# A fused attention and MLP kernel: one attention unit leaves the prologue and is worked through beside the first MLP steps

## The reference

```python
q_d = q.reshape(B, H, Sd, 4, D).mean(axis=3)          # the same for k_d, v_d
out_d = sm_attn(q_d, k_d, v_d)                        # softmax attention, 144 x 144
out_up = np.repeat(out_d, 4, axis=2)
mask = np.abs(pos[:, None] - pos[None, :]) < 4        # local attention
out_local = softmax(where(mask, scale * q @ k.T, -1e9)) @ v
x = (out_up + out_local)                              # 2304 tokens x 512
h = x @ w_in;  x = (h - np.tanh(h)) @ w_out           # 512 -> 2048 -> 512
h = x @ w2_in; out = (h * np.cos(h)) @ w2_out
```

## Time and profile before

| | |
|---|---|
| three runs | 918.26, 919.24 and 924.06 us, median 919.24 |
| the profiled execution | 918.26 us, span from the first to the last instruction 916.1 us |
| TensorE busy in the span | 903.7 us (99%) |
| DVE, ACT, POOL busy | 522.8, 376.0, 146.4 us |
| granted TensorE clock | 1.00 over the span |
| DMA | 59.57 MB, of it 20.45 MB in the first 90 us |

### The profile page before, as it was taken

How to read it: one execution, slowest core, us unless ns; L and a number is a source line. 1 busy time by engine, 2 the same in 40 slices (tenths; PEclk the granted TensorE clock), 3 DMA queues, 4 the chain that set the end, 5 groups by cost and what they waited for, 6 DMA issues and landing times.

```text
span 916.1 us, 15863 instructions
## 1 busy us (share of the span) xinstructions
PE 903.7 (99%) x6264; PEld 838.9 (92%) x6264; DVE 522.8 (57%) x1071; ACT 376.0 (41%) x1055; POOL 146.4 (16%) x167
## 2 busy tenths in 40 slices
PE   8899999999999999999999999999999999999998
PEld 6689999999999999999999999999999999898997
DVE  5733544444445434433334787777777777777775
ACT  6744443443344334422232444443443434443433
POOL 5587400200000100000079820000000000000000
PEclk9999999999999999999999999999999999999999
DMA  9692012821004600301134501001001000000000
GB/s 297 234 297 65 1 58 75 184 71 47 1 34 132 164 1 1 105 1 35 60 114 138 161 1 35 35 1 35 35 1 35 35 1 1 35 1 1 36 1 34
DMA packets 24637, 59.57 MB, mean 65 GB/s; under 512 B 2292, under 2 KB 5492, under 8 KB 24564
## 3 DMA queue, kind: packets, MB, share of 16 engines
q1 hardware_dynamic: 22212, 50.01, 15.9%
q0 software_dynamic: 2352, 8.55, 5.2%
HBM read 49.12 MB, written 9.44 MB: 64 GB/s over the span
## 4 chain that ended last, share of the span: by engine, by line
PE 96%; DMA 2%; DVE 1%; ACT 1%; issue 0%; POOL 0%; POOLq 0%
PE ps L488 44%; PE ps L533 22%; PE ps L514 22%; PE ps L406 2%; DMA qk<-qkx_in 2%; PE ps L446 1%; PE ps L457 1%; PE ps L415 1%; PE ps L389 1%; PE ps L424 1%; PE ps L430 1%; PE ps L401 1%; ACT ps L595 0%; DVE x L789 0%; DVE ps L737 0%
## 5 line engine op out<-in xcount | busy, mean ns | idle before, releaser
L488 PE MATMUL ps<-xh,wi_hi 128*128 128x384 f32 x768 | 261.9, 341 | 2.2 <-DVE gl L830 2.2
L488 PE MATMUL ps<-xh,wi_lo 128*128 128x384 f32 x768 | 258.0, 336 | 0.0
L488 PE MATMUL ps<-xl,wi_hi 128*128 128x384 f32 x768 | 257.3, 335 | 0.0
L488 PEld LDWEIGHTS ps<-xh,wi_hi 128*128 128x128 f32 x768 | 144.2, 188 | 9.4 <-DVE gl L830 2.5
L488 PEld LDWEIGHTS ps<-xl,wi_hi 128*128 128x128 f32 x768 | 144.3, 188 | 4.0
L488 PEld LDWEIGHTS ps<-xh,wi_lo 128*128 128x128 f32 x768 | 144.1, 188 | 0.0
L635 ACT ACTIVATE gh<-rem 128x384 fp32r<-128x384 f32 x96 | 50.5, 526 | 213.6 <-PE ps L533 141.7
L822 DVE TENSOR_TENSOR ps<-ps,fn 128x384 f32<-128x384 f32 x96 | 54.2, 565 | 144.3 <-ACT fn L623 143.4
L514 PE MATMUL ps<-gh,wo_hi 128*128 128x384 f32 x384 | 132.3, 345 | 0.0
L514 PE MATMUL ps<-gl,wo_hi 128*128 128x384 f32 x384 | 128.5, 335 | 0.0
L514 PE MATMUL ps<-gh,wo_lo 128*128 128x384 f32 x384 | 128.4, 334 | 0.0
(11 more groups left out here) (86 smaller groups left out, 1110.3 us busy)
## 6 DMA issues: line engine op xcount, KB each, us to landing
qk<-qkx_in SPq DMA_DIRECT2D x20, 512.0 KB, 4.8
wi_raw<-w_in_in SPq DMA_DIRECT2D x32, 256.0 KB, 5.1
wo_raw<-w_out_in SPq DMA_DIRECT2D x8, 1024.0 KB, 6.0
qkd<-qkf_in POOLq DMA_DIRECT2D x9, 576.0 KB, 7.0
vb<-vx_in SPq DMA_DIRECT2D x20, 256.0 KB, 3.1
y_between<-stage SPq DMA_DIRECT2D x6, 768.0 KB, 3.5
x<-y_between SPq DMA_DIRECT2D x6, 768.0 KB, 5.3
out<-stage SPq DMA_DIRECT2D x18, 256.0 KB, 2.1
```

The lines of the kernel that those rows point to most:

```text
L488: mm = MM(ps[:, h_bank(s), 0:NT], w, xx[:, kc, :], start=(n == 0), stop=(n == last))
```

## The change

Batch 0's last local block, unit 4 before, becomes unit 8. It keeps its own load buffer (buffer 4) and its PSUM pair (`banks` now holds for u <= FIRST). `FIRST` is 8: the prologue takes four local and four pooled units. Unit 8 is scored between the halves of `hidden(0)`, where unit 9 stood; its transposes come ahead of `hidden(2)` and its mixes behind it, ahead of `contract(0)`. Since it sits in banks 0 and 1, `contract(0)` takes banks 2 and 3 first. Its gather now adds to x, and the pooled units' gathers copy for its tokens. Units 9 to 35 are the same as before, each two places later (unit 9 is scored at place 0, unit 10 at place 5). The loads are reordered, the load of unit 10's q and k has left the list written ahead of the loop, and GpSimd issues its first two adding DMAs one block earlier. The filling matmuls are redistributed.

```diff
-UNITS = [("local", 0, n, 0) for n in range(NL)] + [("pooled", 0, i, hs) for hs in range(2) for i in range(2)]
+UNITS = [("local", 0, n, 0) for n in range(4)] + [("pooled", 0, i, hs) for hs in range(2) for i in range(2)] + [("local", 0, 4, 0)]
...
-FIRST = 9
+FIRST = 8
...
-            u, rest = divmod(place + 2 - later, 5)
-            return FIRST + u if u >= (later == 0) and rest == 0 and FIRST + u < NU else None
+            u, rest = divmod(place - later, 5)
+            return FIRST + 1 + u if place >= later and rest == 0 and FIRST + 1 + u < NU else None
...
             load_v(0)
-            load_qk(4)
+            load_qk(FIRST)
             load_v(1)
             load_v(2)
+            load_wi(0, 0, w_in)
             load_v(3)
-            load_v(4)
-            load_wi(0, 0, w_in)
             load_wo(0, 0, w_out)
+            load_v(8)
             load_wi(0, 1, w_in)
...
-            load_qk(FIRST)
+            load_qk(9)
             load_first_of_four(1)
             load_wo(0, 1, w_out)
-            load_v(FIRST)
+            load_v(9)
             load_wi(0, 2, w_in)
-            load_qk(FIRST + 1)
             sp.wait_ge(v_added, after(2))
             load_wo(0, 2, w_out)
-            load_v(FIRST + 1)
             load_wi(0, 3, w_in)
...
-                    for j in range(KC):
+
+                    order = (2, 3, 0, 1) if s == 0 else range(KC)
+                    for j in order:
+                        if s == 0 and j == 2:
+                            pe.wait_ge(gathered, after(FIRST))
                         if s == 0 and j == 0:
-
-                            pe.wait_ge(gathered, after(FIRST))
+                            pe.wait_ge(gathered, after(FIRST + 1))
...
                 attention(2 * s)
+                if s == 0:
+                    transposes(FIRST)
                 hidden(s + AHEAD)
+                if s == 0:
+                    mixes(FIRST)
                 attention(2 * s + 1)
...
-            for u in range(3):
-                sums_of_block(u)
+            sums_of_block(0, 0)
+            sums_of_block(1, 1)
             gp.wait_ge(v_first, 16)
             gp.dma_start(vd[0:QH, :, :].rearrange("p c n -> p (c n)"), v4[0, 2], accum_op=ALU.add).then_inc(v_accumulated, 16)
-            sums_of_block(3)
+            sums_of_block(2, 2)
             gp.wait_ge(v_second, 16)
             gp.dma_start(v_other[0:QH, :], v4[0, 3], accum_op=ALU.add).then_inc(v_accumulated, 16)
-            sums_of_block(4)
+            sums_of_block(3, 3)
+            sums_of_block(FIRST, 4)
```

More of the change, by code:

```diff
@@ L58 @@
 NU = len(UNITS)
-FIRST = 9
+FIRST = 8
 LOCALS = [u for u in range(NU) if UNITS[u][0] == "local"]
 LBUF = {u: 0 for u in LOCALS}
-LBUF[1], LBUF[2], LBUF[3], LBUF[4] = 1, 2, 3, 4
+LBUF[1], LBUF[2], LBUF[3], LBUF[8] = 1, 2, 3, 4
 LAST_POOLED = [max(u for u in range(NU) if UNITS[u][:2] == ("pooled", b)) for b in range(B)]
@@ L196, in banks @@
         def banks(u):
-            return 2 * (u % 4) if u < FIRST else 6
+            return 2 * (u % 4) if u <= FIRST else 6
         def bank_user(u):
@@ L203, in pr_of @@
         def pr_of(u):
-            return pr_first[u % 3] if u < FIRST else pr_all
+            return pr_first[u % 3] if u <= FIRST else pr_all
         def pt_of(u):
-            return pt_first[u % 3] if u < FIRST else pr_all
+            return pt_first[u % 3] if u <= FIRST else pr_all
         def rows_of(u):
@@ L338, in _ @@
             for u in range(FIRST + 1, NU):
-                if 5 * (u - FIRST) - 2 >= 2 * FC * (next_store + 1):
+                if 5 * (u - FIRST - 1) >= 2 * FC * (next_store + 1):
                     store_y(next_store)
@@ L511, in contract @@
                         for n, (w, gg) in enumerate(((hi, g_hi), (lo, g_hi), (hi, g_lo))):
-                            if j == 0 and n == 2:
+                            if j == order[0] and n == 2:
                                 pe.wait_ge(gl_done, after(s + 1))
@@ L535, in contract @@
                         mm.then_inc(o_done, 1)
-            FILL = {0: 7, 1: 2, 2: 6, 3: 1, 4: 1, 5: 1, 6: 2, 7: 2, 8: 2, 9: 2, 10: 3}
-            for k in range(-1, FIRST + 1):
+            FILL = {0: 7, 1: 2, 2: 6, 3: 1, 4: 1, 5: 2, 6: 2, 7: 2}
+            for k in range(-1, FIRST + 2):
                 if k + 1 < FIRST:
@@ L546, in _ @@
                 else:
-                    pe.wait_ge(gathered, after(6))
-                    keep_warm(FILL[k + 1], banks(5))
+                    pe.wait_ge(gathered, after(bank_user(FIRST) + 1))
+                    keep_warm({FIRST - 1: 4, FIRST: 2, FIRST + 1: 3}[k], banks(FIRST))
                 if 0 <= k - 2:
                     mixes(k - 2)
-                if 0 <= k - 1:
+                if 0 <= k - 1 < FIRST:
                     transposes(k - 1)
-            keep_warm(FILL[FIRST + 1], banks(5))
-            mixes(FIRST - 1)
             hidden(0, range(0, 2))
@@ L601, in evacuate @@
                 sc.wait_ge(transposed, after(u + 1))
-                if u < FIRST:
+                if u <= FIRST:
                     sc.wait_ge(mixed, after(u - 2))
@@ L664, in _ @@
                     exponentials(k)
-                if 5 <= k < FIRST:
-                    hi_of_in(0, k - 5)
-                if k == FIRST - 1:
+                if 4 <= k < FIRST:
+                    hi_of_in(0, k - 4)
+                if k == FIRST:
                     split_x(0, 0)
@@ L688, in _ @@
                     exponentials(FIRST)
+                if s == 1 - AHEAD:
+                    evacuate(FIRST)
                 attention(2 * s + 1)
@@ L874, in _ @@
                     normalise(k - 1)
-                if k == FIRST:
-                    split_x(0, 0)
-                    split_x(0, 1)
                 if 0 <= k - 2:
@@ L882, in _ @@
                     maximum(k + 1)
+                if k == FIRST:
+                    split_x(0, 0)
+                    split_x(0, 1)
             split_x(0, 2)
@@ L894, in attention @@
                     maximum(now)
+                    if now == FIRST + 1:
+                        gather(FIRST)
                     guard(now)
@@ L941, in _, with sums_of_block @@
             pieces = iter(range(1, 8 * WG * KC))
-            def sums_of_block(u):
+            def sums_of_block(u, turn):
                 i, n = LBUF[u], UNITS[u][2]
@@ L952, in sums_of_block @@
                     TT(two, four[:, :, :, :, 0], four[:, :, :, :, 1], ALU.add).then_inc(pair_summed, 1)
-                    gp.wait_ge(pair_summed, after(2 * u + hf + 1))
+                    gp.wait_ge(pair_summed, after(2 * turn + hf + 1))
                     TT(qkd[:, :, g0:g0 + gn], two[:, :, :, 0], two[:, :, :, 1], ALU.add).then_inc(qk_summed, 1)
@@ L1030, in _ @@
                 lo_of_in(2, c, 13 + c)
-            gp.wait_ge(mixed, after(FIRST))
+            gp.wait_ge(mixed, after(FIRST + 1))
             split_wo(0, 2)
```

## The result

The changed kernel takes 926.6 us (median of 10 runs, 925.25 to 928.61), the kernel before 921.23 (10 runs, 918.26 to 926.74). The ratio is 1.0057, with an interval of 1.0039 to 1.0075: some 5 us slower, within 1%, and 1.1 us above the top of the predicted range.

What follows compares the result with a forecast made beforehand. TensorE, busy 903.7 of 916.1 us, and what it waits for were taken as the bound. From 918.26 us: -2.7 (prologue and stream), -2.2 (unit 11's wait), +6.5 (unit 10's load), +1.7 (clock) gave 921.5 us, range 914.5 to 925.5.

Steps and rivals of the forecast that it cites:

- the prologue's gain: Attention prologue: one unit's turn fewer, so `hidden(0)` starts at 33.3 instead of 36.56, -3.3 us (-2.0 to -3.6).
- The predicted wait: TensorE at unit 10's scores: q and k load lands at 60.7, due at 54.1, +6.5 us.
- Rival 1: No late load: queue keeps 0.36 MB/us, unit 10's load at most 2 us late; 913.4 to 915.4 us, chance 0.20.
- Unit 11's wait: TensorE's idle time for unit 11's late q and k load disappears, its queue being empty ahead; -2.2 us.
- the mixes: Deferred unit 8's 32 mix matmuls, in the stream behind `hidden(2)`, remain on TensorE's path; +0.65 us.
- A wait that is added: Prologue: unit 4, now pooled, has scores waiting for GpSimd's sums, ending at 17.12; +0.5 to +0.6 us.
- rival 4: Prologue gives 1.5 us less, a q and k load or vd sum being late; 923 us, 0.13 with rival 5.
- ScalarE's wait: Before unit 7's mixes: `split_x` no longer precedes an evacuation that TensorE awaited 0.82 us; -0.8 to -1.1 us.
- the low clock: Behind the wait for unit 10's load, TensorE's clock falls for a spell; +1.7 us, between 0 and 3.4.
- Rival 2: The wait at unit 10's scores comes, but TensorE's clock stays up; 919.9 us, chance 0.17.
- rival 3: Clock falls at unit 10's wait and stays low over 15 us, slower by over 1%; 928 to 932, chance 0.04.
- Rival 5: Change doesn't do what it says, a serialisation in `contract(0)` undoing it; 1 us, 922.5 us, 0.13 with rival 4.

Runs made afterwards that it cites:

- Experiments two: Changed kernel with unit 10's q and k load issued behind the third w_in group, ahead of 3.1 MB of weights; 916.09 us, ratio 0.9953.
- seven: Kernel before with only unit 10's q and k load moved back, behind the last w_out group; 934.6 us, ratio 1.0143.
- the control: The changed kernel run once more, unedited; median 926.55 us, ratio 1.0063, its profiled execution 924.90 us.
- experiment one: Changed kernel with GpSimd's first two adding DMAs one block later, as in the kernel before; 925.31 us, ratio 1.0048.
- the profile after: First profiled execution of the changed kernel, unedited; 929.99 us, longer than each of the ten measured runs.
- experiment eight: Changed kernel with GpSimd's second and third adding DMAs for batch 1 issued later, behind weight splits; 922.27 us, ratio 1.0001.
- experiment ten: Changed kernel with first two adding DMAs one block later, unit 10's q and k load earlier, block 8's ahead of v; 914.61 us, ratio 0.9911.
- experiment nine: Kernel before with unit 10's v load moved to the end of the load list; 922.09 us, ratio 1.0009.
- experiment twelve: Kernel before with five more warming matmuls in the last turns of its prologue; 920.74 us, ratio 0.9994.
- experiment six: Changed kernel with 28 warming matmuls filling the wait ahead of unit 10's scores; 927.42 us, ratio 1.0043, its profiled execution 923.76 us.

## Why the prediction was wrong

**Right: the mechanism and its main term.** I forecast that the prologue's gain would be handed to a DMA. Experiments two and seven show this from both sides: with the load 3.1 MB earlier the changed kernel beats the one before; with it at the end of the list the kernel before loses 12.9 us, there in part through a v load's wait that stood ahead of it. The predicted wait was 6.5 us, the control's is 6.51 (7.0 in experiment one, 9.0 in the profile after). The rate behind it, 0.223 MB/us beside adding DMAs against 0.36 alone, held: from 44.3 us to the landing at 62.65 the control's hardware queue moved 4.03 MB, 0.220 MB/us, and the load landed 19.74 us behind its issue, where "about 20 us" was forecast, and with fewer adds beside it in 17.15 (experiment eight). Rival 1, which let the queue keep its rate, is refuted. The Trainium skill's 358 GB/s as the limit of one core ("DMA: Bandwidth & Descriptors", section Specifications) fits neither stretch of the control: 397 GB/s at 56 to 58 us, when no adding DMA moved data, and 229 at 60 to 62, when one did. The Trainium skill says on the same page, "DMA: Bandwidth & Descriptors", section Queues, rings and completion order, that each DMA engine consumes the descriptors of a ring in order; the trace agrees, with 512 KB behind the weights taking 19.74 us. Unit 11's wait went, the gl wait went but for 0.46 us, the mixes cost what they were put at.

**The step that failed: "A wait that is added".** It let the sums end at 17.12, as before, because "GpSimd's order is otherwise the same work", and put the wait at 0.5 to 0.6 us. Together with the shorter relay that made `hidden(0)` start at 33.3. It came at 35.32 in the control, 2.0 us later, for two reasons.

The larger one, 1.4 us, is the end of the sums. They ended at 18.43 in the control and at 17.29 to 19.65 in the six profiles with this prologue. The work was the same, but GpSimd waited for loads that it had not waited for before: 0.81 us for the target of the first adding DMA in the control (0.69 to 1.54 in four others, none in experiment eight), and with the adds put back 0.75 us for block 8's q and k (experiment one). With the adds late and that load early the sums end at 17.07, and `hidden(0)` starts at 33.95 (ten). This is rival 4's effect, to which I had given, with another, 0.13. Its text had block 8's load there "by 14 to 14.5"; in experiment one it came at 15.7. What share the order of the adding DMAs has in it, and what share the loads' spread from execution to execution, stays open.

The smaller one, 0.65 us, is there with the sums on time too: 33.95 is still later than 33.3. The prediction's own numbers for the wait give 0.64 + 0.62 - 0.43 = 0.83, not 0.5 to 0.6, and experiment ten bears the 0.83 out: transposes(2) start at 18.48 there and at 17.68 before. The rest is the gain of -0.8 to -1.1 on ScalarE's wait, taken at its upper end: -2.76 - 0.8 + 0.83 is -2.7, and ten measured -2.6.

**A term mis-sized: the low clock.** Taken at 1.7 us from seven warming matmuls, it measured 2.9 in the control and 2.1 in the profile after. Its bound of 3.4 held. Rival 2 (the clock stays up) is refuted by the windows at 58 to 68, rival 3 (low for over 15 us) too: it was back within some 7 us of the first matmul.

**A base mis-sized.** The sum was made against 918.26, an execution with the clock at 1.00 throughout and among the lowest seen; I allowed 1 us for "a median taken anew". The median of before was 921.23 beside the result, 3.0 higher, and 920.73 to 922.12 over 17 to 26 runs; from median to median the change cost 5.4 us, where 3.3 was forecast. The changed kernel's median lies 1.65 above its control profile. In the runs of before beside experiment twelve the time goes with the granted clock that each run lists: 918.0 to 919.0 us at 1.000, 923.5 to 925.4 at 0.991 to 0.992. So for the kernel before these are low-clock stretches in some executions; the profiles of experiments seven and nine show one at 34 to 40 us. What triggers them in one execution and not in the next stays open. The changed kernel's 1.65 isn't explained by that: its executions listed at 0.994, the clock of the control's profile (924.90), spread from 923.64 to 928.56. That spread stays open.

Together: 921.5 + 2.0 + 1.2 is 924.7, against 924.90 for the control's profiled execution; another 1.65 makes its median, 926.55. The range's top of 925.5 held about the upper ends of the wait (8) and of the clock (3.4), which give 924.8, and most of the 1 us for the median, but a start of `hidden(0)` at its forecast only: the control's gain of 1.2 us lies outside the stated 2.0 to 3.6. Rival 5 fell: the order did what it says.

## What to carry to other kernels

In a queue that works in order, a load's landing is set by all the bytes and all the waits in front of it: when steps move, walk the queue again by bytes, with the rate of the stretch (here 0.22 MB/us beside adding DMAs), before counting the gain of the step. The wait of 6.5 us cost 9.4 with the clock that it let fall, and one line that moved 0.5 MB ahead of 3.1 MB of weights brought some 10. An instruction put earlier in an in-order engine needs its own inputs' landing looked up, even when it only issues a DMA; and a sum should start from a median and a range that adds its errors up.

## What was unexpected in the hardware

How long TensorE may stand still before its clock falls had no single answer here. 2.17 us left the matmuls behind at full speed in the profile before, and so did 1.51 in experiment nine; 1.78 us at the pooled scores left the control at 1.00, while in experiment six 1.43 us in the same place were followed by 0.52. 2.45 us, in the place of the 2.17 and in nearly the same kernel, left the matmuls at half: in TensorE's timeline of experiment twelve the 32 score matmuls take 1.97 us, not 1.15.

```profile
68.29 0.69 PE L401 MATMUL ps<-mask_r,eye_r 128*128 128x256 f32 x2 [2.45 <-DMA qk<-qkx_in]
68.91 1.97 PE L406 MATMUL ps<-qk 64*64 64x64 f32 x32
```

The cost of a fall hardly grew with the wait: scores and `contract` behind it took 6.14 us after 4.4 us of waiting, 6.69 after 6.5, 5.89 after 9.0 and 5.57 after 14.3, against 3.83 at full speed. The Trainium skill, "TensorE: Matmul & The Clock Gate", section HAM oscillation, tells of waits for DMAs between bursts of matmuls that send the gate back to half rate; the trace agrees at every wait of 2.45 us and more that was not filled.
